# The first batch of an attention phase: another order of projections, gates and token splits

## The chip, the cores and the metric

The kernel runs on one NeuronCore of one Trainium2 chip. The metric is the device time of one execution in microseconds (us). The core has five engines with a queue of instructions each: TensorE (PE, matrix products into PSUM), VectorE (DVE), ScalarE (ACT), GpSimd (POOL) and SyncE (SP, here only DMA issues). Each queue runs in order; semaphores tie the queues together.

## The reference, cut to what matters

Eight batches of 576 tokens pass through linear attention and an MLP (the first phase, three quarters of the time) and then through a small mixture of attention experts (the second phase), of which this is the whole computation for a batch `x` (576 x 512):

```python
logits = x @ w_gate                              # 4 experts
topk = the two largest; w = softmax over those two
for e in range(4):
    q, k, v = x @ wq[e], x @ wk[e], x @ wv[e]     # head width 64
    scores = q @ k.T / 8, causal mask
    a = softmax(scores)
    out += (w of e where e is chosen, else 0) * (a @ v @ wo[e])
```

## The kernel before, in words

Every fp32 operand of a projection is split into a high part that TensorE multiplies fast (`hi`, a rounding cast) and the rest (`lo = x - hi`), and each product is three: hi*hi, lo*hi, hi*lo. So `Y[n]` holds a batch's tokens as `y_hi` and `y_lo`, alternately in two buffers, and each PSUM result that is an operand again is taken out twice: ScalarE casts the high part (`fill_hi`), then VectorE subtracts (`fill_lo`).

A batch of the second phase has these pieces of work:

- `("M", m)`, m = 0..7: the queries and keys of expert pair `p = m // 4` and half `h` of the sequence (`project_m`, 12 products, 256 columns wide for h = 0 and 320 for h = 1). m even is queries, odd is keys.
- `("V", t)`, t = 0..4: values and gate logits of a tile of 128 tokens (`project_v`, 12 products of 260 columns). ScalarE copies the values, VectorE the logits.
- 18 units (`UNITS`), 9 per expert pair: one head by 128 queries. `scores(n)` makes two units, and is called for two such pairs at steps 0, 4, 9 and 13, and alone at 8 and 17. `masked` (VectorE) adds the mask, writes the row to SBUF and finds the row maximum (`nmax`); `exponentials` (ScalarE) follows; `over_sum` (VectorE, L1351 and L1353) inverts the row sums; `scale` (GpSimd) multiplies by that and the gate; `turn_blocks` (VectorE, L1358) transposes blocks; `write_turned` (SP, four DMAs) and `land` (issued by ScalarE, which first waits for those four) carry the result through memory; `weighted` (TensorE) multiplies with the values.
- `("OUT", t)`: the product with `wo`, in the next batch.
- gates: `gates(st, shift, part)`, parts 0, 1 and 2 on VectorE (2, 6 and 10 small instructions), an exponential on ScalarE between (`gate_exp`).
- the split of the tokens two batches ahead: `load_y` (SP), `split_y` (GpSimd: four high parts and four low parts, alternating).

All engines walk the same 18 steps of a batch in their own queue, each doing its part of the step. `FILL` says which projection TensorE does in step n as filling between scores, `WEIGH` in which step `weighted` stands (steps from 18 on belong to the next batch), `TWOS` how units are grouped in twos. A step's fill goes to one of two PSUM banks (`bank(n)`), so it waits until the fill two before has been taken out (`fill_before`, `evacuated`). `scores(n)` waits for the maxima of the units that had its bank before: `scores(0)` of a batch waits for unit 16 of the batch before, `scores(2)` for unit 17.

Before step 0 of the very first batch there is a list, `ORDER0`: V0 to V3, M0 to M3, V4. The first batch then fills M4 to M7 (steps 0 to 3), V0 to V4 of batch 1 (4 to 8), M0 (9), M1, M2, M3 of batch 1 (15 to 17). Its gates stand in steps 0, 1 and 2, the gates of batch 1 in steps 14, 15 and 17 (`GATES_AT`). GpSimd makes batch 1's tokens (`split_y(.., 1, n)`) before its step 0, those of batch 2 from step 5 on, and splits `wo` in step 13 (L818, L820). VectorE's queue in a step is written out so:

```python
if n < UNITS and second(n, last):
    masked(st, n, first, last)
if fill_at(n - 1, first, last):
    fill_lo(...)
if n < UNITS and not second(n, last):
    masked(st, n, first, last)
```

and after these `sums_lo`, `over_sum` for the two units that began at n - 1, `turn_blocks` for those that began at n - 3, and the gates.

Of the kernel before, what the change touches and what calls it, by code (L numbers as in the profile page):

```python
# [5 lines left out]
ALU = mybir.AluOpType  # L6
# [10 lines left out]
def plain(ap):  # L17

    return ap.bitcast(F32)


def program(nc, q, k, v, g_ln, w_ch1, w_ch2, w_gate, wq, wk, wv, wo, out):
# [35 lines left out]
    with ExitStack() as ctx:  # L58
# [203 lines left out]
        for n in range(NT):  # L262
            FILL[4 + n] = ("V", n)
            FILL[10 + n] = ("OUT", n)

        WEIGH = {11: [(0, 0)], 17: [(0, 1)], UNITS + 2: [(1, 0)], UNITS + 8: [(1, 1)]}

        TWOS = [[p * NS + u for u in us] for p in range(EP) for us in ((0, 1), (2, 3), (4, 5), (6, 7), (8,))]
# [7 lines left out]

        def fill_at(n, first, last):

            if n == -1:
                return None if first else (("M", 3), 0)  # L280
            f = FILL.get(n)
            if f is None or (f[0] == "OUT" and first) or (last and (f[0] == "V" or (f[0] == "M" and f[1] < 4))):
                return None
            return f, {"OUT": -1, "V": 1, "M": 0 if f[1] >= 4 else 1}[f[0]]

        def fill_before(n, first, last):

            for at in range(n - 2, -1, -2):
                if fill_at(at, first, last):
                    return fill_at(at, first, last)  # L290
            return ((("M", 3), ("V", NT - 1))[n % 2] if first else ("M", 2 + n % 2)), 0

# [31 lines left out]

        def weighed(n, first, last):
            if last:
                own = [(w, 0) for w in WEIGH_LAST.get(n, [])]
            else:
                own = [(w, 0) for w in WEIGH.get(n, [])] if n < UNITS else []
            return own + ([] if first else [(w, -1) for w in WEIGH.get(n + UNITS, [])])  # L330

# [63 lines left out]

        ORDER0 = [("V", 0), ("V", 1), ("V", 2), ("V", 3), ("M", 0), ("M", 1), ("M", 2), ("M", 3), ("V", 4)]

# [19 lines left out]
        w2_in, wo_in_s = sem("w2_in"), sem("wo_in_s")  # L417
        w2s_hi, w2s_lo = sem("w2s_hi"), sem("w2s_lo")
        y0hi_a, y0lo_v, wo_g = sem("y0hi_a"), sem("y0lo_v"), sem("wo_g")
        y_ld = [sem(f"y_ld{kt}") for kt in range(KT)]  # L420
# [99 lines left out]
        def _(sp_):  # L520
# [153 lines left out]
            def batch(st, first=False, last=False, more=True):  # L674
                if more:
                    need2(sp_, "ylo_g", st, 1, KT)
                    load_y(st, 2)
                for n in range(UNITS):
                    f = fill_at(n - 1, first, last)
                    if f and f[0][0] == "OUT":  # L680
                        out_store(st, -1, f[0][1])
                    for k, shift in twos_at(n, 3, first, last):
                        if not (last and shift == 0):
                            write_turned(st, shift, k)
# [17 lines left out]
        def _(pool):  # L702
# [74 lines left out]
            def split_y(st, shift, n):  # L777
# [7 lines left out]
                else:  # L785
                    need2(pool, "yhi_g", st, shift, kt + 1)
                    pool.tensor_tensor(to[1][:, kt, 0:S], y_in[:, kt, :], plain(to[0][:, kt, 0:S]), ALU.subtract).then_inc(sems["ylo_g"], 1)

            def scale(st, shift, k, last):

                turn = last and shift == 0
                if k == 0:
                    need2(pool, "gate_v", st, shift, PER["gate_v"])
                need2(pool, "rrec_v", st, shift, 2 * k + 2)
                if not turn:
                    nth = nth_turned(st, shift, k)
                    if nth >= 4:
                        pool.wait_ge(px_out[nth % 4], 64 * (nth // 4))
                for i, u in enumerate(units_of(k, turn)):
                    p, s = unit(u, turn)  # L800
                    t = TILES_OF[s]
                    x = to = PR[s][:, 0 : P * t]
                    if not turn:

                        x = x.rearrange("p (j b c) -> p j b c", b=4, c=32)
                        to = PX[nth % 4][:, 0 : blocks_of(k)].rearrange("p (b x) -> p b x", b=4)[:, :, i * t * 32 : (i + 1) * t * 32].rearrange("p b (j c) -> p j b c", c=32)
                    g = G[(st[1] + shift) % 2][:, p, s : s + 1]
                    pool.tensor_scalar(to, x, rrec[:, 1, u : u + 1], g, ALU.mult, ALU.mult).then_inc(sems["pscale_g"], 1)  # L808

            def batch(st, first=False, last=False, more=True):  # L810
                for n in range(UNITS + 1 if last else UNITS):
                    for k, shift in twos_at(n, 2, first, last):
                        scale(st, shift, k, last)
                    if more and 5 <= n < 5 + 2 * KT:
                        split_y(st, 2, n - 5)
                    if first and n == 13:
                        pool.wait_ge(wo_in_s, 16 * E)
                        pool.tensor_tensor(WO[0][:], wo_in[:], ones[:, 0:1].rearrange("p (a c) -> p a c", a=1).to_broadcast([P, EP, D]), ALU.mult).then_inc(wo_g, 1)  # L818
                        pool.wait_ge(wo_g, 1)
                        pool.tensor_tensor(WO[1][:], wo_in[:], plain(WO[0][:]), ALU.subtract).then_inc(wo_g, 1)  # L820

            pool.sem_inc(sems["yhi_g"], KT)
            pool.sem_inc(sems["ylo_g"], KT)
            for n in range(2 * KT):
                split_y((0, 0), 1, n)
            batch((0, 0), first=True)
# [7 lines left out]
        def _(act):  # L834
# [135 lines left out]
            def gate_exp(st, shift):  # L970
                need2(act, "gate_v", st, shift, 2)
                act.activation(gate[:], gate[:], ACT.Exp).then_inc(sems["gexp_a"], 1)

            def exponentials(st, n, last):
                s = unit(n, last)[1]
                w = keys_of(s)
                need2(act, "nmax_v", st, 0, n + 1)
                act.activation(PR[s][:, 0:w], PR[s][:, 0:w], ACT.Exp, bias=nmax[:, n : n + 1], scale=-1.0, accum_out=rsum[:, n : n + 1]).then_inc(sems["exp_a"], 1)  # L978

            def batch(st, first=False, last=False):  # L980
                for n in range(STEPS_LAST if last else UNITS):
                    if n < UNITS and second(n, last):
                        exponentials(st, n, last)
                    if fill_at(n - 1, first, last):
                        f, shift = fill_at(n - 1, first, last)
                        fill_hi(st, shift, f, bank(n - 1))
                    for w, shift in weighed(n - 1, first, last):
                        sums_hi(st, shift, w, first, last and shift == 0)
# [11 lines left out]
                    if n < UNITS and not second(n, last):  # L1000
                        exponentials(st, n, last)
                    if n == 0 and first:
                        gate_exp(st, 0)
                    if n == GATES_AT[1] and not last:
# [5 lines left out]
            for i, f in enumerate(ORDER0):  # L1010
                if i == 1:
                    need(act, "y_v", (PAIRS, 0), KT)
                    act.copy(Y[0][0][:, :, CW:S], ysb[:, 0, :, 0:TAIL]).then_inc(y0hi_a, 1)
                if f == ("M", 0):
                    act.wait_ge(const2_g, 2)
                fill_hi((0, 0), 0, f, bank0(i))
            batch((0, 0), first=True)
            for n in range(1, 5):
# [8 lines left out]
        def _(dve):  # L1027
# [356 lines left out]
            def batch(st, first=False, last=False):  # L1384
                for n in range(STEPS_LAST if last else UNITS):
                    if n < UNITS and second(n, last):
                        masked(st, n, first, last)
                    if fill_at(n - 1, first, last):
                        f, shift = fill_at(n - 1, first, last)
                        fill_lo(st, shift, f, bank(n - 1))  # L1390
                    if n < UNITS and not second(n, last):
                        masked(st, n, first, last)
                    for w, shift in weighed(n - 1, first, last):
                        sums_lo(st, shift, w, last and shift == 0)
                    for k, shift in twos_at(n, 1, first, last):
                        over_sum(st, shift, k, last)
                    for k, shift in twos_at(n, 3, first, last):
                        if not (last and shift == 0):
                            turn_blocks(st, shift, k)
                    if first and n < 3:  # L1400
                        gates(st, 0, n)
                    if not last and n in GATES_AT:
# [17 lines left out]
            dve.wait_ge(const2_v, 1)  # L1420
            dve.wait_ge(const2_g, 13)
            batch((0, 0), first=True)
            for n in range(1, 5):
# [6 lines left out]
        def _(pe):  # L1430
# [251 lines left out]
            def batch(st, first=False, last=False):  # L1682
                for n in range(STEPS_LAST if last else UNITS):
# [5 lines left out]
                    if last and lagging(n, T_LAG, True, last):  # L1689
                        transposes(st, lagging(n, T_LAG, True, last)[0])  # L1690
                    for w, shift in weighed(n, first, last):
                        weighted(st, shift, w, first and shift == 0, last and shift == 0)
                    if fill_at(n, first, last):
                        f, shift = fill_at(n, first, last)
                        what, x = f
                        held, when = fill_before(n, first, last)
                        evacuated(st, when, held)
# [21 lines left out]
            for i, f in enumerate(ORDER0):  # L1719
# [5 lines left out]
                if i == 0:  # L1725
                    pe.wait_ge(y0lo_v, KT)
                if f == ("M", 2):
                    pe.wait_ge(y0lo_v, KT + 1)
                if f == ("V", NT - 1):
                    pe.wait_ge(const2_v, 1)  # L1730
# [37 lines left out]
```

## Time and profile before

| | |
|---|---|
| median of three runs | 1256.91 us (1255.25 to 1259.26) |
| the profiled execution: its own time | 1256.5 us |
| its span, first to last instruction | 1254.7 us |
| mean granted TensorE clock | 0.995 of full |
| second phase, from its first projection | 891.6 us on |
| first batch, steps 0 to 17 | about 905 to 948 us |

The rows below give a start in us from the beginning of the span and a duration. A clock of 1.00 is TensorE's level of 2.4 GHz, a stretch of about 0.5 is its level of 1.2 GHz.

### The profile page before, as it was taken

The numbers are of one execution on the slowest core, as the hardware profiler recorded it, in microseconds if no ns is written. First come the engines' busy times: TensorE is split into PE (matmuls) and PEld (weight loads), VectorE is DVE, ScalarE is ACT, GpSimd is POOL, SyncE is SP. The second block draws the span as 40 slices with busy tenths as digits, with TensorE's granted clock in tenths as the row PEclk, the third lists the DMA queues.
The fourth block names the chain that finished last, engine by engine and source line by source line (L and its number), as shares of the span: only waits on it lengthen the run. The fifth ranks groups of instructions, "written<-read, shape, count | busy, mean of one in ns | idle before, by whom it ended". The sixth has DMA issues, their size and how long they took to land.

```text
span 1254.7 us, 19440 instructions
## 1 busy us (share of the span) xinstructions
PE 1223.0 (97%) x7136; PEld 1016.7 (81%) x7136; DVE 668.7 (53%) x1750; ACT 379.5 (30%) x858; POOL 224.3 (18%) x252
## 2 busy tenths in 40 slices
PE   8989999999999999999999999999988999999998
PEld 7878888888888888888888888888977788878876
DVE  5785365465365375365365313311476666666652
ACT  4462131131131131131131111111334455445545
POOL 3532000000000000000000000001474455445321
PEclk9999999999999999999999999999989999999989
DMA  8741550550460360370370130250356777786742
GB/s 183 179 105 46 130 78 9 124 86 5 121 95 5 107 110 5 103 112 5 92 123 5 45 90 7 67 112 1 89 149 175 222 207 209 220 234 195 188 128 76
DMA packets 344735, 133.05 MB, mean 106 GB/s; under 512 B 240960, under 2 KB 329024, under 8 KB 344640
## 3 DMA queue, kind: packets, MB, share of 16 engines
q1 hardware_dynamic: 296400, 108.85, 36.3%
q10 hardware_dynamic: 48240, 22.94, 7.3%
q8 instruction: 58, 0.95, 0.3%
q14 instruction: 37, 0.30, 0.1%
HBM read 72.10 MB, written 42.86 MB: 92 GB/s over the span
## 4 chain that ended last, share of the span: by engine, by line
PE 79%; DVE 9%; DMA 3%; ACT 3%; SPq 3%; issue 2%; ACTq 0%; POOL 0%; DVEq 0%; POOLq 0%
PE hb L1434 31%; PE yb L1522 30%; PE sc L1434 9%; PE pa L1451 3%; DMA turned<-px 3%; PE ob L1678 2%; DVE px L1358 2%; ACT prob L978 1%; SPq L672 1%; DVE prob L1376 1%; PE pa L1442 1%; PE sc L1644 1%; SPq L531 1%; DVE k_lo L1295 1%; DMA vsb<-in_v_dram 0%
## 5 line engine op out<-in xcount | busy, mean ns | idle before, releaser
L1228 DVE SCALAR_TENSOR_TENSOR hid_lo<-hb,hid_hi 128x512 fp32r<-128x512 f32 x144 | 99.4, 690 | 383.3 <-ACT hid_hi L868 383.3
L868 ACT ACTIVATE hid_hi<-hb 128x512 fp32r<-128x512 f32 x144 | 85.8, 597 | 614.8 <-PE hb L1434 614.8
L1522 PE MATMUL yb<-hid_hi,w_hi 128*128 128x512 f32 x576 | 226.5, 393 | 2.4 <-DVE hid_lo L1228 2.4
L1434 PE MATMUL hb<-xn_hi,w_hi 128*128 128x512 f32 (+1 forms) x580 | 228.2, 393 | 0.0
L1434 PE MATMUL hb<-xn_lo,w_hi 128*128 128x512 f32 (+1 forms) x580 | 225.2, 388 | 0.0
L1434 PE MATMUL hb<-xn_hi,w_lo 128*128 128x512 f32 (+1 forms) x580 | 225.0, 388 | 0.0
L1522 PE MATMUL yb<-hid_hi,w_lo 128*128 128x512 f32 x576 | 224.3, 389 | 0.0
L1522 PE MATMUL yb<-hid_lo,w_hi 128*128 128x512 f32 x576 | 224.1, 389 | 0.0
L1434 PEld LDWEIGHTS hb<-xn_hi,w_hi 128*128 128x128 f32 x580 | 108.9, 188 | 25.7 <-issue 2.3
L1522 PEld LDWEIGHTS yb<-hid_hi,w_hi 128*128 128x128 f32 x576 | 108.1, 188 | 24.9 <-issue 2.8
L1434 PEld LDWEIGHTS hb<-xn_hi,w_lo 128*128 128x128 f32 x580 | 108.9, 188 | 22.8
L1522 PEld LDWEIGHTS yb<-hid_hi,w_lo 128*128 128x128 f32 x576 | 108.1, 188 | 22.8
L1434 PEld LDWEIGHTS hb<-xn_lo,w_hi 128*128 128x128 f32 x580 | 109.0, 188 | 21.3
L1522 PEld LDWEIGHTS yb<-hid_lo,w_hi 128*128 128x128 f32 x576 | 108.2, 188 | 21.7
L978 ACT ACTIVATE prob<-prob,nmax 128x128 f32<-128x128 f32 (+3 forms) x144 | 84.0, 584 | 124.8 <-DVE nmax L1376 109.6
L808 POOL TENSOR_SCALAR px<-prob,rrec,g 128x128 f32<-128x128 f32 (+4 forms) x126 | 79.5, 640 | 146.1 <-DVE rrec L1353 130.4
L716 POOL TENSOR_TENSOR vsb<-ones 128x40 f32<-128x40 f32 x8 | 2.4, 306 | 507.6 <-PE hb L1434 507.6
L1434 PE MATMUL sc<-y_hi,wqk_hi 128*128 128x256 f32 (+1 forms) x256 | 79.5, 310 | 8.3 <-DVE k_lo L1295 4.8
L1434 PE MATMUL sc<-y_lo,wqk_hi 128*128 128x256 f32 (+1 forms) x256 | 75.8, 296 | 0.0
L1434 PE MATMUL sc<-y_hi,wqk_lo 128*128 128x256 f32 (+1 forms) x256 | 75.8, 296 | 0.0
L1434 PEld LDWEIGHTS sc<-y_hi,wqk_hi 128*128 128x128 f32 x256 | 48.7, 190 | 14.0 <-DVE k_lo L1295 6.2
L1358 DVE STREAM_TRANSPOSE px<-px 128x256 f32<-128x256 f32 (+4 forms) x70 | 57.9, 828 | 0.0
(221 smaller groups left out, 1853.1 us busy)
## 6 DMA issues: line engine op xcount, KB each, us to landing
qx<-in_q_dram SPq DMA_DIRECT2D x32, 288.0 KB, 5.5
ksb<-in_k_dram SPq DMA_DIRECT2D x8, 1024.0 KB, 5.7
vsb<-in_v_dram SPq DMA_DIRECT2D x32, 256.0 KB, 4.8
stage<-in_moe_w_ch_dram SPq DMA_DIRECT2D x16, 512.0 KB, 3.9
xn_lo<-ksb SPq DMA_DIRECT2D x128, 64.0 KB, 2.0
y_scratch<-ysb SPq DMA_DIRECT2D x32, 256.0 KB, 2.9
ysb<-xsb SPq DMA_DIRECT2D x128, 64.0 KB, 2.1
out_dram<-osb SPq DMA_DIRECT2D x32, 256.0 KB, 4.2
```

The lines of the kernel that those rows point to most:

```text
L531: sp_.dma_start(qx[b * 32 : (b + 1) * 32], q_v[st[1], st[0], b // 2, b % 2]).then_inc(q_in, 16)
L672: sp_.dma_start(to[a], PX[nth % 4][a * 32 : (a + 1) * 32, 0 : 4 * w].rearrange("c (b x) -> c b x", b=4)).then_inc(px_out[nth % 4], 16)
L808: pool.tensor_scalar(to, x, rrec[:, 1, u : u + 1], g, ALU.mult, ALU.mult).then_inc(sems["pscale_g"], 1)
L868: act.activation(HID[f % 2][0][:], hb[f % 2][:], ACT.Relu).then_inc(sems["hhi_a"], 1)
L978: act.activation(PR[s][:, 0:w], PR[s][:, 0:w], ACT.Exp, bias=nmax[:, n : n + 1], scale=-1.0, accum_out=rsum[:, n : n + 1]).then_inc(sems[" ...
L1228: dve.scalar_tensor_tensor(out=lo[:], in0=hb[f % 2][:], scalar=0.0, in1=plain(hi[:]), op0=ALU.max, op1=ALU.subtract).then_inc(sems["hlo_v" ...
L1295: dve.tensor_tensor(K[1][:, p, s0 * HQ : s1 * HQ], src[:, 0 : CHUNK[h]], plain(K[0][:, p, s0 * HQ : s1 * HQ]), ALU.subtract).then_inc(sems ...
L1358: dve.transpose(x, x).then_inc(sems["px_v"], 1)
L1434: ins = pe.matmul(dst, l, r, start=(n == 0), stop=(n == len(terms) - 1))
L1451: ins = pe.matmul(dst[r, X_BANK[g], g % 2 * 2 * (HD + 1) : (g % 2 + 1) * 2 * (HD + 1)], qx[:, g, 4 * t : 4 * t + ROWS[t] // 32, :], KV[:, ...
L1522: ins = pe.matmul(yb[j][:], l, r, start=(f == 0 and m == 0 and not first), stop=(f == FT - 1 and m == 2), skip_group_check=True)
L1678: ins = pe.matmul(OB[nth % 2][e * HD : (e + 1) * HD, at : CHUNK[h]].rearrange("p (a c) -> p a c", c=32), v[:, j, 2 * p + e, :], PT[h][:, a ...
```

## The change

`ORDER0` becomes M0, M1, V0 to V4. The first batch gets tables of its own: M2 and M3 in steps 0 and 1, M4 to M7 in 2 to 5, V0 to V4 of batch 1 in 6 to 10, M0 and M1 of batch 1 in 11 and 12, M2 and M3 in 16 and 17. The weighted sums of its second half of queries (0, 1) move from step 17 to step 1 of batch 1. Gates parts 0 and 1 stand before step 0, part 2 in step 1 ahead of the fill. The high parts of batch 1's tokens are cast by ScalarE (`y1_hi`: one before the batch, three in steps 0 to 2), GpSimd does the low parts only (`y1_lo`: one before, two in step 2, one in step 4). GpSimd's split of batch 2's tokens starts in step 9, the split of `wo` moves to step 17, and SP's loads of batch 2's tokens go to step 4.

```diff
+        FILL_FIRST = {n: (("M", 2 + n), 0) for n in range(6)}
+        FILL_FIRST.update({6 + n: (("V", n), 1) for n in range(NT)})
+        FILL_FIRST.update({(11, 12, 16, 17)[n]: (("M", n), 1) for n in range(4)})
+
         WEIGH = {11: [(0, 0)], 17: [(0, 1)], UNITS + 2: [(1, 0)], UNITS + 8: [(1, 1)]}
+        WEIGH_FIRST = {11: [(0, 0)], UNITS + 1: [(0, 1)], UNITS + 2: [(1, 0)], UNITS + 8: [(1, 1)]}
...
-            return ((("M", 3), ("V", NT - 1))[n % 2] if first else ("M", 2 + n % 2)), 0
+            return (("V", 3 + n % 2) if first else ("M", 2 + n % 2)), 0
...
-        ORDER0 = [("V", 0), ("V", 1), ("V", 2), ("V", 3), ("M", 0), ("M", 1), ("M", 2), ("M", 3), ("V", 4)]
+        ORDER0 = [("M", 0), ("M", 1), ("V", 0), ("V", 1), ("V", 2), ("V", 3), ("V", 4)]
...
             def batch(st, first=False, last=False, more=True):
-                if more:
-                    need2(sp_, "ylo_g", st, 1, KT)
-                    load_y(st, 2)
                 for n in range(UNITS):
+                    if more and n == (4 if first else 0):
+                        need2(sp_, "ylo_g", st, 1, KT)
+                        load_y(st, 2)
...
+            def y1_lo(kt):
+
+                pool.wait_ge(y1hi_a, kt + 1)
+                pool.tensor_tensor(Y[1][1][:, kt, 0:S], y_in[:, kt, 0:S], plain(Y[1][0][:, kt, 0:S]), ALU.subtract).then_inc(sems["ylo_g"], 1)
...
-                    if more and 5 <= n < 5 + 2 * KT:
-                        split_y(st, 2, n - 5)
-                    if first and n == 13:
+                    if first and n in (2, 4):
+                        for kt in ((1, 2), (3,))[n // 4]:
+                            y1_lo(kt)
+                    at = n - (9 if first else 5)
+                    if more and 0 <= at < 2 * KT:
+                        split_y(st, 2, at)
+                    if first and n == UNITS - 1:
...
-            for n in range(2 * KT):
-                split_y((0, 0), 1, n)
+            y1_lo(0)
...
+            def y1_hi(kt):
+                act.wait_ge(y_ld[kt], 32)
+                act.copy(Y[1][0][:, kt, 0:S], y_in[:, kt, 0:S]).then_inc(y1hi_a, 1)
...
-                    if n == 0 and first:
-                        gate_exp(st, 0)
+                    if first and n < KT - 1:
+                        y1_hi(n + 1)
...
+            y1_hi(0)
+            gate_exp((0, 0), 0)
+            act.wait_ge(const2_g, 2)
             batch((0, 0), first=True)
...
                         masked(st, n, first, last)
+                    if first and n == 1:
+                        gates(st, 0, 2)
...
-                    if first and n < 3:
-                        gates(st, 0, n)
...
+            gates((0, 0), 0, 0)
+            gates((0, 0), 0, 1)
             batch((0, 0), first=True)
```

## Rows read from the trace of the kernel before

**Rows 1.** The page's first line: the span.

```profile
span 1254.7 us, 19440 instructions
```

**Rows 2.** Windows: stretch, length, busy time (PE, PEld, DVE, ACT, POOL), TensorE clock, DMA.

```profile
905.20:918.00 12.80, 10.52 (x74) 9.05 (x73) 9.01 (x37) 5.47 (x17) 7.28 (x7) 0.87 0.28 93
914.50:918.50 4.00, 4.00 (x21) 2.92 (x20) 2.57 (x14) 1.59 (x6) 1.24 (x3) 0.57 0.48 173
918.00:954.70 36.70, 28.88 (x217) 24.96 (x217) 27.68 (x92) 14.85 (x48) 24.80 (x26) 0.95 0.60 157
...
954.70:1207.50 252.80, 248.97 (x1835) 209.42 (x1836) 168.51 (x639) 124.69 (x386) 119.18 (x150) 1.00 0.74 207
```

**Rows 3.** The chain that ended last: the second phase's first projections (V0, V1).

```profile
891.58 2.89 PE ob L1434 x24
```

**Rows 4.** TensorE's timeline: the first instruction of ten pieces; idle before, releaser.

```profile
897.21 0.28 PE L1434 MATMUL sc<-y_hi,wqk_hi 128*128 128x256 f32 x1
...
900.03 0.31 PE L1434 MATMUL sc<-y_hi,wqk_hi 128*128 128x320 f32 x1
...
903.56 0.39 PE L1434 MATMUL sc<-wvg_hi,y_hi 128*128 128x260 f32 x1
...
906.09 0.39 PE L1434 MATMUL sc<-y_hi,wqk_hi 128*128 128x256 f32 x1
...
913.13 0.42 PE L1434 MATMUL sc<-y_hi,wqk_hi 128*128 128x320 f32 x1 [2.28 <-DVE k_lo L1295]
...
917.91 0.47 PE L1434 MATMUL sc<-wvg_hi,y_hi 128*128 128x260 f32 x1
...
933.68 0.50 PE L1644 MATMUL sc<-k_hi,q_hi 64*128 64x512 f32 x2 [2.36 <-DVE nmax L1376]
...
941.56 2.27 PE L1678 MATMUL ob<-pt,v 128*64 128x320 f32 x20 [1.23 <-DMA pt<-turned]
...
946.38 0.41 PE L1434 MATMUL sc<-y_hi,wqk_hi 128*128 128x320 f32 x1 [2.55 <-DVE k_lo L1295]
...
958.41 0.44 PE L1644 MATMUL sc<-k_hi,q_hi 64*128 64x384 f32 x2
```

**Rows 5.** Timeline of GpSimd and VectorE: two pairs that overlap.

```profile
910.33 1.43 POOL L787 TENSOR_TENSOR y_lo<-y_in,y_hi 128x576 fp32r<-128x576 f32 x1
...
910.53 1.33 DVE L1327 TENSOR_TENSOR gcmp<-gcmp,before 128x80 f32<-128x80 f32 x1
...
939.10 2.43 POOL L820 TENSOR_TENSOR wo_lo<-wo_in,wo_hi 128x1024 fp32r<-128x1024 f32 x1
...
939.95 1.62 DVE L1323 TENSOR_TENSOR gate<-logit,gmx 128x20 f32<-128x20 f32 x1
```

**Rows 6.** VectorE's timeline: V4's logits, gates (first and last), two of the masks.

```profile
905.71 0.16 DVE L1307 COPY logit<-sc 128x4 f32<-128x4 f32 x1 [1.01 <-ACT v L936]
...
909.29 1.06 DVE L1325 TENSOR_TENSOR gcmp<-logit 128x80 f32<-128x80 f32 x1
...
912.44 0.17 DVE L1330 TENSOR_SCALAR grank<-grank 128x20 f32<-128x20 f32 x1
...
913.33 0.17 DVE L1333 TENSOR_TENSOR gate<-gate,grank 128x20 f32<-128x20 f32 x1
...
914.47 0.67 DVE L1343 COPY g<-gate 32x2 f32<-32x2 f32 x4
...
928.49 0.29 DVE L1376 CUSTOM_DVE_ANT_0 prob<-tb,mask 128x128 f32<-128x128 f32 x1
...
944.06 0.69 DVE L1376 CUSTOM_DVE_ANT_0 prob<-sc,mask 128x512 f32<-128x512 f32 x1
```

**Rows 7.** ScalarE's timeline: four token casts, a pair of query casts, an exponential.

```profile
886.67 2.17 ACT L1009 CAST y_hi<-y_in 128x512 fp32r<-128x512 f32 x4
...
902.26 0.42 ACT L932 CAST qt_hi<-sc 64x64 fp32r<-64x64 f32 x2
...
907.50 0.39 ACT L978 ACTIVATE prob<-prob,nmax 128x128 f32<-128x128 f32 x1
```

More of the change, by code:

```diff
@@ L275, in program, with fill_at @@
         STEPS_LAST = UNITS + 5
-        def fill_at(n, first, last):
+        def fill_at(n, st, first, last):
             if n == -1:
                 return None if first else (("M", 3), 0)
+            if first:
+                f = FILL_FIRST.get(n)
+                return None if f is None else f
             f = FILL.get(n)
@@ L284, in fill_at, with fill_before @@
             return f, {"OUT": -1, "V": 1, "M": 0 if f[1] >= 4 else 1}[f[0]]
-        def fill_before(n, first, last):
+        def fill_before(n, st, first, last):
             for at in range(n - 2, -1, -2):
-                if fill_at(at, first, last):
-                    return fill_at(at, first, last)
-            return ((("M", 3), ("V", NT - 1))[n % 2] if first else ("M", 2 + n % 2)), 0
+                if fill_at(at, st, first, last):
+                    return fill_at(at, st, first, last)
+            return (("V", 3 + n % 2) if first else ("M", 2 + n % 2)), 0
         def lagging(n, lag, first, last):
@@ L323, in landing, with weighed @@
             return PT[h][:, at : at + (4 if u == NS - 1 else 8), 0:t, :]
-        def weighed(n, first, last):
+        def weighed(n, st, first, last):
             if last:
@@ L328, in weighed @@
             else:
-                own = [(w, 0) for w in WEIGH.get(n, [])] if n < UNITS else []
-            return own + ([] if first else [(w, -1) for w in WEIGH.get(n + UNITS, [])])
+                own = [(w, 0) for w in (WEIGH_FIRST if first else WEIGH).get(n, [])] if n < UNITS else []
+            return own + ([] if first else [(w, -1) for w in (WEIGH_FIRST if st[1] == 1 else WEIGH).get(n + UNITS, [])])
         def unit(n, turn):
@@ L418, in program @@
         w2s_hi, w2s_lo = sem("w2s_hi"), sem("w2s_lo")
+        y1hi_a = sem("y1hi_a")
         y0hi_a, y0lo_v, wo_g = sem("y0hi_a"), sem("y0lo_v"), sem("wo_g")
@@ L674, in batch @@
             def batch(st, first=False, last=False, more=True):
-                if more:
-                    need2(sp_, "ylo_g", st, 1, KT)
-                    load_y(st, 2)
                 for n in range(UNITS):
-                    f = fill_at(n - 1, first, last)
+                    if more and n == (4 if first else 0):
+                        need2(sp_, "ylo_g", st, 1, KT)
+                        load_y(st, 2)
+                    f = fill_at(n - 1, st, first, last)
                     if f and f[0][0] == "OUT":
@@ L820, in batch @@
                         pool.tensor_tensor(WO[1][:], wo_in[:], plain(WO[0][:]), ALU.subtract).then_inc(wo_g, 1)
-            pool.sem_inc(sems["yhi_g"], KT)
+            pool.sem_inc(sems["yhi_g"], 2 * KT)
             pool.sem_inc(sems["ylo_g"], KT)
-            for n in range(2 * KT):
-                split_y((0, 0), 1, n)
+            y1_lo(0)
             batch((0, 0), first=True)
@@ L983, in batch @@
                         exponentials(st, n, last)
-                    if fill_at(n - 1, first, last):
-                        f, shift = fill_at(n - 1, first, last)
+                    if fill_at(n - 1, st, first, last):
+                        f, shift = fill_at(n - 1, st, first, last)
                         fill_hi(st, shift, f, bank(n - 1))
-                    for w, shift in weighed(n - 1, first, last):
+                    for w, shift in weighed(n - 1, st, first, last):
                         sums_hi(st, shift, w, first, last and shift == 0)
@@ L1013, in _ @@
                     act.copy(Y[0][0][:, :, CW:S], ysb[:, 0, :, 0:TAIL]).then_inc(y0hi_a, 1)
-                if f == ("M", 0):
-                    act.wait_ge(const2_g, 2)
                 fill_hi((0, 0), 0, f, bank0(i))
+            y1_hi(0)
+            gate_exp((0, 0), 0)
+            act.wait_ge(const2_g, 2)
             batch((0, 0), first=True)
@@ L1387, in batch @@
                         masked(st, n, first, last)
-                    if fill_at(n - 1, first, last):
-                        f, shift = fill_at(n - 1, first, last)
+                    if first and n == 1:
+                        gates(st, 0, 2)
+                    if fill_at(n - 1, st, first, last):
+                        f, shift = fill_at(n - 1, st, first, last)
                         fill_lo(st, shift, f, bank(n - 1))
@@ L1392, in batch @@
                         masked(st, n, first, last)
-                    for w, shift in weighed(n - 1, first, last):
+                    for w, shift in weighed(n - 1, st, first, last):
                         sums_lo(st, shift, w, last and shift == 0)
@@ L1690, in batch @@
                         transposes(st, lagging(n, T_LAG, True, last)[0])
-                    for w, shift in weighed(n, first, last):
+                    for w, shift in weighed(n, st, first, last):
                         weighted(st, shift, w, first and shift == 0, last and shift == 0)
-                    if fill_at(n, first, last):
-                        f, shift = fill_at(n, first, last)
+                    if fill_at(n, st, first, last):
+                        f, shift = fill_at(n, st, first, last)
                         what, x = f
-                        held, when = fill_before(n, first, last)
+                        held, when = fill_before(n, st, first, last)
                         evacuated(st, when, held)
@@ L1726, in _ @@
                     pe.wait_ge(y0lo_v, KT)
-                if f == ("M", 2):
+                if f == ("V", NT - 1):
                     pe.wait_ge(y0lo_v, KT + 1)
-                if f == ("V", NT - 1):
                     pe.wait_ge(const2_v, 1)
```

## The prediction

> **What bounds the kernel now.** I read the views from the outside in. The profiled execution took 1256.5 us, of which 1254.7 are its span [rows 1] and 1.8 lie around it; the median of the runs, 1256.91, is 0.4 above it. The change touches only the second phase's first batch, so I cut the phase into windows [rows 2]. From 954.70 to 1207.50 TensorE is busy 248.97 of 252.80 us at full clock, and the change leaves that stretch's instructions alone: whatever the first batch saves or loses arrives at the end undiminished. In the first batch and the start of the second, TensorE stands still 12.80 - 10.52 = 2.3 us and 36.70 - 28.88 = 7.8 us, and its clock is short by 12.80 x 0.13 = 1.7 and 36.70 x 0.05 = 1.8 us. That makes 13.6 us, the most that any order can win.
>
> TensorE's timeline says whom it waited for [rows 4]: VectorE, three times out of four. Once it is a low part that stood behind the gates (M7 at 913.13, 2.28 us late, after which the clock fell to 0.57 for 4 us [rows 2]), once a row maximum (933.68, 2.36), once a low part again (946.38, 2.55), and once a DMA (941.56, 1.23). So the question for each edit is what it does to VectorE's queue.
>
> **The opening.** Before, V0 starts at 891.58 [rows 3], and four V take until 897.21: 1.41 each. M0 and M1 take 900.03 - 897.21 = 2.82, M2 and M3 903.56 - 900.03 = 3.53, V4 and the first two scores 2.53 together, and M4 starts at 906.09 [rows 4]. After, the order is M0, M1, five V, scores, M2, M3: the same work, so M4 could start at 906.1 again. What changes is when VectorE and ScalarE get their input: scores(0) starts at 891.58 + 2.82 + 5 x 1.41 = 901.5, about 3.5 us earlier.
>
> M4 needs M2's bank, so M2's low part. Before it on VectorE stand, from V4's logits on, gates parts 0 and 1, two masks and part 2. V4's logits were there 905.87 - 903.56 = 2.3 after V4's start [rows 4, 6]; after, that is 900.05 + 2.3 = 902.3. Part 0 is two instructions of the kind of L1330 and L1333 (0.2 each with the gap): 0.4. Part 1 took 912.61 - 909.29 = 3.3 before [rows 6], in which L1325 (1.06) and L1327 (1.33) are far above their neighbours of about 0.2; without these excesses it is 1.3 to 1.4. Here it meets the first `y1_lo` on GpSimd, 1.43 us [rows 5]. I take 902.3 + 0.4 + 1.3 + 1.4 = 905.4 (904.0 without the meeting). Two masks of 0.3, then part 2, 915.14 - 913.33 = 1.8 [rows 6]: 907.9. On ScalarE from 905.8: exp(0) 0.5 with its read-out, `y1_hi(1)` 2.17 / 4 = 0.54 for 512 columns, so 0.6 for 576, exp(1) 0.5, M2's casts 0.3 + 0.4 [rows 7]: 908.1. Then VectorE's low part of M2 with its turned queries, 0.8: M4 starts near 909.1, 3.0 us later than before, and the clock falls as it did after the 2.28 us. From M4 to V0 of batch 1 TensorE had 917.91 - 906.09 - 2.28 - 1.7 = 7.9 us of work; with one clock loss of 1.7 again, V0 starts at 909.1 + 7.9 + 1.7 = 918.7 against 917.91. So the old stall before M7 is not removed: it moves ahead to M4 and grows a little, because two thirds of the gates stand in front of the first maxima instead of between them. Loss here 0.8; if gates meet no GpSimd instruction, gain 0.6.
>
> **Token work.** Four high parts leave GpSimd for ScalarE, 0.6 us each on an engine that is busy 5.47 of 12.80 us [rows 2]; their cost is only the one or two that stand before M2's casts, counted above. If ScalarE had no slack, all four would cost 2.4. The last low part follows scale(1) in step 4, near 916, ahead of V0's 918.7; that is its cover, 2 us. SP's loads of batch 2 wait for it and then finish near 922; GpSimd wants them in step 9, near 925.
>
> **Steps 6 to 17.** TensorE runs V0 to V4, scores and M0, M1 of batch 1 nearly without a wait. With S(9) two fills earlier, the mask of unit 9 comes at 928.49 - 2 x 1.4 + 0.8 = 926.5 or a little before: 926.0 to 926.5. From here VectorE's and ScalarE's chain of maxima, exponentials, sums and transposes governs. Before, it took from 928.49 to 944.06, 15.6 us, for units 9 to 16 [rows 6]. After, it holds in addition a logit and a low part (0.5), and the neighbours on GpSimd differ. A VectorE instruction with SBUF operands only that meets a GpSimd instruction ends when that ends: L1327 at 911.86 behind `y_lo` at 911.76, L1323 at 941.57 behind `wo_lo` at 941.53 [rows 5], where their like take 0.2. The change lays GpSimd's eight token splits into steps 9 to 16, that is beside the gates of batch 1 (steps 14, 15), where before only `wo` stood. I expect three meetings on the path, of 1.1 to 1.4 by these rows, 3.7 in all: L1351, and L1326 and L1328 or their neighbours. The stretch before holds such meetings too (L1323's 1.4 is in its 15.6), so the net is between -3.7 (none is left) and +4.7 (below); I add 0.7, half a meeting. So unit 16's maximum is there at 926.2 + 15.6 + 0.5 + 0.7 + 0.7 (its own time) = 943.7.
>
> The Trainium skill, page "SBUF — State Buffer", section "Who interferes with whom", states it as a rule: a VectorE instruction with two SBUF inputs and a GpSimd instruction that reads SBUF exclude each other for the whole instruction, while ScalarE waits for neither. The trace agrees with the first half, as the two pairs above show. By the rule the casts moved to ScalarE are free of it; had the meetings shared the port instead of excluding each other, the maximum would come about 3 us sooner.
>
> TensorE has no work until then. Clean work from V0 to the common point (scores(4) of batch 1, 958.41 [rows 4]) is 958.41 - 917.91 - 7.8 - 1.8 = 30.9 us. Of it 10.4 stand behind scores(0) of batch 1: scores 0.9, M4 to M7 2.82 + 3.53, the moved sums (0, 1) 2.27, and (1, 0) at 8/20 of that, 0.9. So TensorE is through at 918.7 + 20.5 = 939.2 and waits 4.5 us for unit 16 at 943.7, then 3.1 for unit 17 at 947.2 (exp(16) 0.8, M2's two casts and two subtractions 1.5, transposes 0.9, the mask 0.7, less overlap). The moved sums would have filled this, but they now stand behind the wait; their old DMA wait of 1.23 and the 2.55 before M3 are gone. From 947.2 remain 10.0 us of work and one clock loss of 1.7: scores(4) at 958.9, 0.5 later than before.
>
> **The sum.** Losses after: 3.0 and 4.5 + 3.1 of standing still and twice 1.7 of clock, 14.0, against 13.6 before, so about +0.5. Carried forward piece by piece with the same durations, the order of before reaches 960.7 where the trace has 958.41, and the order of after 959.5; like for like this says -1.2. I take a value between, nearer to the second: -0.9 from the median, 1256.0. Nothing later changes it [rows 2]. The split of `wo` in step 17, whose second half takes 2.43 [rows 5], holds up gates part 2 at most that long; behind these on VectorE wait M3's low part and the first masks of batch 1, and M4 and the sums (0, 1), 3.7 us, cover it. Uncovered it costs up to 2.4.
>
> **Rivals.**
> - *The meetings stay away (faster).* VectorE's gates fall between GpSimd's instructions. For it: part 2 of the first gates, ten instructions in 1.8 us [rows 6], ran without a meeting. Against: GpSimd's scale is released by `over_sum`, and the splits follow at once, so they return beside the same VectorE instructions. Unit 16 comes 3.7 earlier: 1252.3. Chance 0.19. Less than 941 for scores(0) of batch 1 decides it.
> - *Every wait of the first batch goes (faster still).* The work is there; against it is all of VectorE's queue. -9 to -13: 1246. Chance 0.03.
> - *Every port-bound instruction of the gates meets one (slower).* Part 0, part 1 and L1351 have seven; each 1.2 is 8.4 instead of the 3.7 on the path: +4.7, 1260.7. GpSimd has four splits in that stretch, 1.43 or a little less each, the scales between and `wo` after it, so the supply is there. Chance 0.10. It decides if scores(2) of batch 1 start after 951.
> - *The opening goes as meant* (M4 without a wait): 4.7 us are won by V0, but the chain of maxima starts only as much earlier as VectorE is free, and the clock stays up: 1253 to 1255, inside the forecast's range. It is a part of the forecast's case.
>
> **How the numbers follow.** Forecast as told: 0.68. About 0.3%, 3.8 us, is what a measurement of this kernel tells from no change, so faster means under 1253.1 and slower over 1260.7. Faster 0.22 is the sum of the first two rivals; slower 0.10; same 0.68. The range reaches to 1251.0, which leaves about 1 in 10 of the faster cases and the 1246 outside, and up to 1260.3, short of the slower rival.
>
> **What would show it.** M4 of the first batch starts near 909 with about 3 us of idle time, released by M2's low part (`qt_lo`), and a clock near 0.57 in the next 4 us; V0 of batch 1 near 918.7. No stall over 1 us between 919 and 938. Then one stall of 3 to 5 us and one of 2 to 4 before scores(0) and scores(2) of batch 1, released by `nmax`, with L1323, L1326 or L1328 over 1 us beside `y_hi`, `y_lo`. Scores(4) of batch 1 within 956 to 961. The forecast is wrong if the scores of batch 1 start without a wait, or if the chain of maxima is short enough in its own right.

## The result, and the profile after

The changed kernel takes 1260.97 us (median of 14 runs, 1256.62 to 1262.35), the kernel before 1257.03 (14 runs, 1254.92 to 1260.51). The ratio is 1.0029, with a 95% interval of 1.0018 to 1.0040: slower, by 3.9 us in the medians. That is 0.7 us above the range. The prediction put the bound of "slower" at about 0.3%, or 1260.7 us: the median is just over the second, the ratio just under the first.

The profiled execution after has a span of 1260.3 us, 5.6 more than before. Its second phase starts 1.2 us later (892.77 instead of 891.58, [rows 3]) in a stretch that the change does not touch, so 4.4 are the phase's own. I count times from that first projection below ("+x"). The windows of after, with the columns of [rows 2]:

```profile
905.20:918.00 12.80, 10.28 (x76) 9.48 (x75) 8.92 (x41) 7.56 (x26) 6.46 (x8) 1.00 0.05 11
918.00:954.70 36.70, 22.96 (x172) 20.34 (x171) 26.77 (x84) 12.63 (x40) 23.36 (x24) 0.85 0.66 183
954.70:970.00 15.30, 15.30 (x113) 12.92 (x112) 7.75 (x29) 5.98 (x20) 4.00 (x7) 0.92 0.52 131
```

The second window holds the loss: TensorE is idle for 13.7 us instead of 7.8, at a mean clock of 0.85 instead of 0.95. The low clock reaches into the third window (0.92). The steady batches behind it are as full as before: from 970.00 to 1215.00 TensorE is busy 241.05 of 245.00 us, at 1.00. TensorE's timeline after, first instructions of six pieces, against [rows 4]:

```profile
892.77 0.28 PE L1459 MATMUL ob<-y_hi,wqk_hi 128*128 128x256 f32 x1
...
910.11 0.39 PE L1459 MATMUL sc<-y_hi,wqk_hi 128*128 128x256 f32 x1 [2.52 <-DVE qt_lo L1325]
...
918.48 0.39 PE L1459 MATMUL sc<-wvg_hi,y_hi 128*128 128x260 f32 x1
...
951.90 0.47 PE L1669 MATMUL sc<-k_hi,q_hi 64*128 64x128 f32 x2 [10.65 <-POOL wo_lo L839]
...
956.34 2.70 PE L1703 MATMUL ob<-pt,v 128*64 128x320 f32 x20
...
965.09 0.44 PE L1669 MATMUL sc<-k_hi,q_hi 64*128 64x384 f32 x2
```

One row stands out: scores(0) of batch 1 waited 10.65 us, and the releaser is not VectorE's maximum but GpSimd's split of `wo`. In the code that is `pe.wait_ge(wo_g, 2)`, which stands in TensorE's queue between the first batch and the loop over batches 1 to 4 (line 1737 of the kernel before). It cost nothing while the split was made in step 13: [rows 5] have it done at 941.53, and scores(0) of batch 1 started about 948. In step 17 it is behind scale(8). VectorE and GpSimd after, with the meetings (a VectorE instruction that lies beside one of GpSimd and ends when that ends):

```profile
904.06 1.43 POOL L802 TENSOR_TENSOR y_lo<-y_in,y_hi 128x576 fp32r<-128x576 f32 x1 [11.42 <-ACT y_hi L994]
...
904.15 1.43 DVE L1348 TENSOR_TENSOR gcmp<-logit 128x80 f32<-128x80 f32 x1
...
940.59 1.11 DVE L1348 TENSOR_TENSOR gcmp<-logit 128x80 f32<-128x80 f32 x1
...
941.88 1.32 DVE L1350 TENSOR_TENSOR gcmp<-gcmp,before 128x80 f32<-128x80 f32 x1
...
943.99 0.69 DVE L1399 CUSTOM_DVE_ANT_0 prob<-sc,mask 128x512 f32<-128x512 f32 x1
...
947.52 0.76 DVE L1399 CUSTOM_DVE_ANT_0 prob<-tb,maskt 128x576 f32<-128x576 f32 x1
...
948.20 1.26 DVE L1356 TENSOR_TENSOR gate<-gate,grank 128x20 f32<-128x20 f32 x1
...
949.51 2.34 POOL L839 TENSOR_TENSOR wo_lo<-wo_in,wo_hi 128x1024 fp32r<-128x1024 f32 x1
...
949.71 2.16 DVE L1358 TENSOR_SCALAR gmx<-gmx 128x5 f32<-128x5 f32 x1
```

Unit 16's maximum was there at 944.7 and unit 17's at 948.3. Without the wait, scores(0) could have started at 944.7 and scores(2) at 948.3, where they came at 951.9 and 952.6.

### The profile page after: what moved, and what is told of

Same layout as the page of the kernel before. It is cut to its first block, busy times and chain, and to the rows that moved or that the text cites. A ratio compares the mean times of both kernels' runs of the same rounds, so it can differ in the third digit from the quotient of the medians.

```text
span 1260.3 us, 19439 instructions
## 1 busy us (share of the span) xinstructions
PE 1222.0 (97%) x7136; PEld 1017.4 (81%) x7136; DVE 670.2 (53%) x1750; ACT 382.1 (30%) x862; POOL 220.4 (17%) x248
## 4 chain that ended last, share of the span: by engine, by line
PE 77%; DVE 9%; DMA 4%; ACT 3%; SPq 3%; issue 2%; POOL 1%; ACTq 1%; DVEq 0%; POOLq 0%
PE hb L1459 31%; PE yb L1547 30%; PE sc L1459 7%; DMA turned<-px 3%; PE pa L1476 3%; PE ob L1703 2%; DVE px L1381 2%; SPq L682 2%; ACT prob L1000 1%; PE pa L1467 1%; DVE prob L1399 1%; SPq L541 1%; ACTq L986 1%; DVE k_lo L1318 1%; PE sc L1669 1%
## 5 line engine op out<-in xcount | busy, mean ns | idle before, releaser
L1459 PE MATMUL sc<-y_hi,wqk_hi 128*128 128x320 f32 (+1 forms) x248 | 77.2, 311 | 6.5 <-DVE qt_lo L1325 2.5
L1459 PE MATMUL sc<-y_lo,wqk_hi 128*128 128x320 f32 (+1 forms) x248 | 73.3, 296 | 0.0
L1459 PE MATMUL sc<-y_hi,wqk_lo 128*128 128x320 f32 (+1 forms) x248 | 73.3, 296 | 0.0
```

What stands on the lines that cost most here:

```text
L1459: ins = pe.matmul(dst, l, r, start=(n == 0), stop=(n == len(terms) - 1))
```

## The experiments

All ratios are to the kernel before, run in the same group of runs on the same chip, with their 95% intervals. The groups are e1 to e4 (kernel before 1256.75 us), e5 to e8 (1255.96), and e9 and e10 (1256.25). The kernel before differs by up to 0.8 us between groups, so across groups the ratios count and not the medians. Each kernel has 11 or 12 runs, e10 only 6.

**e1: the wait alone.** TensorE waits for `wo` where it is first read.

```diff
             batch((0, 0), first=True)
-            pe.wait_ge(wo_g, 2)
             for n in range(1, 5):
...
                         else:
+                            if x == 0 and st == (0, 1):
+                                pe.wait_ge(wo_g, 2)
                             output(st, shift, x, bank(n), 4 if x == 0 else 0)
```

> The changed kernel with one wait moved: TensorE waits for the split of wo ahead of the first product with wo (step 10 of batch 1), no longer ahead of batch 1's scores(0). Theory (the wait is the loss): scores(0) of batch 1 then start when unit 16's maximum is there, at 944.7 instead of 951.9 in the trace of after, scores(2) at 948.3 instead of about 952.4; the end moves forward by 3 to 4.5 us, so about 1256.5 where the changed kernel has 1261, level with the kernel before or up to 1 us under it. Rival (the wait hides behind VectorE): gates part 2 of batch 1 lasts until 953.1 beside the split of wo and stands ahead of M3's low part and the masks, so TensorE stops at M5 instead and the end moves by less than 1 us: 1260 to 1261.

Measured: 1256.28 us, ratio 0.9991 (0.9978 to 1.0004). The whole loss is gone, with all the rest of the change in place, as the theory had it. TensorE's timeline of e1 (its first projection is at 893.30):

```profile
944.04 0.33 PE L1669 MATMUL sc<-k_hi,q_hi 64*128 64x128 f32 x2 [3.79 <-DVE nmax L1399]
...
947.54 0.58 PE L1669 MATMUL tb<-k_hi,q_hi 64*128 64x256 f32 x2 [2.75 <-DVE nmax L1399]
```

The two stalls that the prediction had (4.5 and 3.1) are here, 3.79 and 2.75, both for row maxima; M5 did not stall. Scores(0) come at +50.7 instead of +59.1 after, scores(4) of batch 1 (959.70) at +66.4 instead of +72.3; before it was +66.8. Of the 8.4 us that scores(0) gain, 5.9 are left at scores(4), in part because the stall before scores(2) is back. The rival, that VectorE's gates part 2 would hold TensorE up as long, is refuted.

A caution for single profiles: the mask that finds unit 16's maximum starts at +51.2 in the changed kernel, +49.9 in e1 and +50.0 in e5, whose instructions are the same up to there. So differences of up to 1.3 us in such a place are scatter, and the medians decide.

**e2: the split of `wo` back in step 13**, the wait where it was (`if first and n == UNITS - 1:` becomes `n == 13`).

> The changed kernel with the split of wo back in step 13; TensorE's wait stays where it was. Theory (the late split is the loss): no wait for GpSimd at batch 1, but 4.3 us of split ahead of scale(7) and between token splits, beside VectorE's gates: 1257 to 1259, so most of the loss gone. Rival (port meetings of VectorE with GpSimd are the loss, the wait only covers them): the meetings in steps 14 and 15 become more, unit 16's maximum comes later than 944, and the time stays at 1260 to 1262.

Measured: 1256.87 us, 1.0003 (0.9989 to 1.0017). The loss is gone this way too, the time a shade under the theory's 1257. The rival (meetings, not the wait) is out: there are more meetings here (L1346 takes 1.62 us beside `wo_lo`), and the loss is gone all the same. They may cost something: scores(0) of batch 1 wait 5.19 us for their maximum and stand at +53.1, 2.4 us after e1's, more than the scatter.

**e3: the kernel before with this one part of the change**, the split of `wo` in step 17.

> The kernel before with one part of the change alone: the split of wo in step 17 instead of 13. Theory (TensorE's wait at the head of batch 1 for a split in step 17): scale(7) ends near 948 there, wo near 952.5, TensorE waits for it from about 948 on, the end is 2 to 4.5 us later: 1259.5 to 1261.5. Rival (the loss comes of the new order, not of wo): within 1 us of the kernel before, 1256 to 1258, because VectorE's queue is relieved in steps 14 and 15 by as much.

Measured: 1259.00 us, 1.0017 (1.0001 to 1.0034). One line gives part of the loss in the old order, half a microsecond less than I had expected at the least, and the interval all but reaches 1. The timeline of e3, in which the split ends at 950.02:

```profile
950.07 0.33 PE L1644 MATMUL sc<-k_hi,q_hi 64*128 64x128 f32 x2 [4.15 <-POOL wo_lo L820]
```

The wait is 4.15 us here and 10.65 in the changed kernel, since there TensorE had been through with steps 16 and 17 long before, and the weighted sums (0, 1) stood behind the wait instead of in front of it. Part of it is paid back: M3's stall is 0.65 in e3, 2.55 before [rows 4].

**e4: the split of `wo` in step 6**, the wait where it was (`n == 6`).

> The changed kernel with the split of wo in step 6, where GpSimd stands idle for 1.8 and 2.7 us around its scales; the wait stays. Theory (late split is the loss): no wait for GpSimd at batch 1, gates part 2 without the meetings of 1.3 and 2.2 us: 1255.5 to 1257.5, the best of these four, since unit 16's maximum stays at 944 to 945. Rival (VectorE's meetings in steps 14 to 17 and its chain are the loss): scores(0) of batch 1 still late by 3 us or more against its chain, 1259 or more.

Measured: 1256.80 us, 0.9999 (0.9986 to 1.0012): in the theory's range, with the rival's 1259 or more out, but not the best of the four. Gates part 2 took its short form (L1356 and L1358 0.17 us each); the meetings of part 1 stayed (L1348 1.10, L1350 1.32), so scores(0) of batch 1 still waited 3.60 and scores(2) 2.96 for maxima, and the split in step 6 delayed the units behind it: scores(11) waited 1.67.

**e5: the moved sums between the two scores.** e1, with `weighted(0, 1)` behind scores(0) of batch 1 and ahead of scores(2). The call is skipped where it stood before; that line is left out here.

```diff
-        WEIGH_FIRST = {11: [(0, 0)], UNITS + 1: [(0, 1)], ...
+        WEIGH_FIRST = {11: [(0, 0)], UNITS: [(0, 1)], ...
...
                         scores(st, n, first, last)
+                        if st == (0, 1) and n == 0:
+                            weighted(st, -1, (0, 1), False, False)
                         if not last and n % NS < NS - 1:
                             scores(st, n + 2, first, last)
```

> The changed kernel with TensorE's wait for wo at its first use, and the moved weighted sums (0, 1) between scores(0) and scores(2) of batch 1 instead of behind both. Theory (TensorE's idle time at the head of batch 1 can be filled by them, only their place behind the wait kept them out): the stall before scores(2), 2.75 us with the wait moved alone, shrinks to about 0.4 and the end comes 1.5 to 2.3 us sooner than that kernel's 1256.3, so 1254 to 1255. Rival (VectorE decides there: gates part 2, lengthened by the split of wo, stands before M3's low part, for which M5 waits): the idle time only moves to M5, 1256 to 1256.5.

Measured: 1254.87 us, 0.9990 (0.9978 to 1.0002), against e1's 0.9991: no difference that these runs can tell, as the rival had it. The median as such lies in the theory's range (1254 to 1255), but that is the faster group and no gain on e1. The trace sides with the rival: the stall before scores(2) (2.75) is gone, new ones of 2.40 before M5 and 0.60 before M6 stand in its place, and scores(4) come at +66.5, where e1 has +66.4. M5 waits for M3's low part behind gates part 2:

```profile
950.73 0.39 PE L1459 MATMUL sc<-y_hi,wqk_hi 128*128 128x256 f32 x1 [2.40 <-DVE k_lo L1318]
```

**e6: the first batch's gates back in steps 0, 1 and 2**, on e1: the calls of `gates` and `gate_exp` as in the kernel before.

> The changed kernel with the wait for wo at its first use, and the first batch's gates back in steps 0, 1 and 2. Theory A (the gates ahead of the first masks cause the 2.5 us stall before M4, but the chain of maxima in steps 9 to 17 decides the end): M4 starts with under 1 us of idle time, a stall of 1 to 2.5 comes back before M6 or M7, and the end stays within 1 us of 1256.3. Theory B (the opening's stall and its clock loss are paid in full): 1252.5 to 1254.5.

Measured: 1257.27 us, 1.0015 (1.0001 to 1.0029). Theory B is out: without the 2.5 us stall before M4 (0.76 here) nothing was won. Theory A's end came true, just (1.0 us above 1256.3), but not its stall of 1 to 2.5 before M6 or M7: small ones came instead (0.60, 0.39, 0.88, and later 1.27). Scores(0) of batch 1 stand at +52.7, 2.0 later than in e1, not much beyond the scatter. The intervals of e6 and e1 overlap by a hair, so that gates ahead of the first masks help a little is likely, not certain.

**e7: the token splits of batch 2 three steps earlier**, on e1 (`at = n - (6 if first else 5)`).

> The changed kernel with the wait for wo at its first use, and GpSimd's split of batch 2's tokens in steps 6 to 13 instead of 9 to 16. Theory (VectorE's gate instructions of batch 1 are held up by these splits, 1.1 and 1.3 us at L1348 and L1350): both take about 0.24 us, unit 16's maximum and scores(0) of batch 1 come 1.5 to 2.2 us sooner, the end 1 to 2.2 us sooner: 1254 to 1255.3. Rival (the waiting time is only moved: over_sum and others meet the splits in the steps before, and ScalarE's waits for the DMAs set the pace): L1348 and L1350 short, but the same end within 0.7 us of 1256.3.

Measured: 1253.06 us, 0.9976 (0.9966 to 0.9986): faster than the kernel before. The median is 0.9 under the theory's range; by the ratios the gain on e1 is 0.15% or 1.9 us, which is in it. The intervals of e7 and e1 overlap (0.9978 to 0.9986), so a gain on e1 is likely, not certain. The rows that the theory named, VectorE and TensorE of e7 (first projection at 890.78):

```profile
938.27 0.24 DVE L1348 TENSOR_TENSOR gcmp<-logit 128x80 f32<-128x80 f32 x1
...
938.69 0.24 DVE L1350 TENSOR_TENSOR gcmp<-gcmp,before 128x80 f32<-128x80 f32 x1
```

```profile
940.57 0.33 PE L1669 MATMUL sc<-k_hi,q_hi 64*128 64x128 f32 x2 [1.42 <-DVE nmax L1399]
```

The same instructions took 1.10 and 1.32 us in e1. Of these 2.0 us, 0.9 arrive at scores(0) (+49.8 against +50.7) and at scores(4) (+65.5 against +66.4), which is within the scatter; scores(2) still wait 2.95. Two more profiles have the early splits, e9 and e10. In e7, e9 and e10 the mask of unit 16 starts at +49.0, +47.9 and +48.3, in the changed kernel, e1 and e5 at +51.2, +49.9 and +50.0. So the maximum does come earlier, by about 1 us at the least.

How much of that reaches the end is not settled, for two other things differ by as much. The mean granted clock over e7's twelve runs is 0.9948, over e1's 0.9927: over 1250 us that is 2.6 us more at full speed. And in the profiles the stretch behind scores(4) of batch 1, in which e1 and e7 have the same instructions, takes 297.5 us in e1 and 294.4 in e7.

**e8: three edits together**, on e1: the sums of e5, the gates of e6, the split of `wo` in step 8.

> A candidate: the changed kernel with the wait for wo at its first use, the sums (0, 1) between scores(0) and scores(2) of batch 1, the first batch's gates back in steps 0 to 2, and the split of wo in step 8. If the idle stretches add up as the single edits suggest: 1252.5 to 1254.5, faster than both kernels. If the chain of maxima through steps 9 to 17 decides alone: 1255.5 to 1256.5.

Measured: 1255.20 us, 0.9994 (0.9979 to 1.0008), between the two ranges and near the second; the single edits do not add up: scores(0) of batch 1 waited 4.49 us for unit 16's maximum, and the sums could not fill that, since they stand behind it.

**e9: `wo` without the port meeting.** e7, and ScalarE casts `wo`'s high part in step 3, GpSimd makes the low part in step 4.

```diff
+                    if first and n == 3:
+                        act.wait_ge(wo_in_s, 16 * E)
+                        act.copy(WO[0][:], wo_in[:]).then_inc(wo_g, 1)
...
-                    if first and n == UNITS - 1:
+                    if first and n == 4:
                         pool.wait_ge(wo_in_s, 16 * E)
-                        pool.tensor_tensor(WO[0][:], wo_in[:], ...
                         pool.wait_ge(wo_g, 1)
```

> A candidate on top of the kernel with the wait at its first use and the token splits in steps 6 to 13: ScalarE casts the high part of wo in step 3, GpSimd makes only its low part, in step 4. Theory (gates part 2 of batch 1 is held up 1.0 and 2.0 us by the split of wo at L1356 and L1358; behind it wait M3's low part and the masks of batch 1): part 2 takes 1.8 us instead of 5, but M5 of batch 1 was covered by M4 and the sums (0, 1), so the end moves little: 1252 to 1253.5, within 1 us of that kernel's 1253.1. Rival (part 2 was on the path of batch 1's maxima): 1250.5 to 1251.5.

Measured: 1254.39 us, 0.9986 (0.9976 to 0.9996). The rival is out. Gates part 2 is short (L1358 and L1360, the lines that were L1356 and L1358, take 0.18 and 0.17 us), and the end does not move forward for it, as expected of something that TensorE's other work had covered. Against e7 it is if anything 1 us worse, inside the intervals, and 0.9 us above the theory's range.

**e10: e9 with the sums of e5.**

> The same candidate with the sums (0, 1) between scores(0) and scores(2) of batch 1. With gates part 2 short, M5 no longer waits for it, so the 2.3 us of sums should now fill the stall of 2.95 before scores(2) for good: 1.5 to 2.3 us under the same kernel without this edit, 1250 to 1251.5. Rival (some later wait takes it back, as in the kernel with this edit alone, where M5 waited 2.4 us): within 0.7 us of it.

Measured: 1251.98 us, 0.9969 (0.9955 to 0.9982), 2.4 us under e9 in the medians of the same group. The gain is slightly more than the theory's 1.5 to 2.3; the time itself is 0.5 us above its 1251.5. All six runs lie under e9's median. It is the fastest kernel of this study, 4.3 us under the kernel before and, by the ratios, about 7.5 under the changed one. TensorE of e10 (first projection at 892.41):

```profile
941.52 0.33 PE L1671 MATMUL sc<-k_hi,q_hi 64*128 64x128 f32 x2 [1.42 <-DVE nmax L1401]
...
945.03 0.39 PE L1671 MATMUL tb<-k_hi,q_hi 64*128 64x256 f32 x2 [0.75 <-DVE nmax L1401]
```

Scores(4) of batch 1 (954.03) are at +61.6, 5.2 us ahead of the kernel before and 3.3 ahead of e9 (+64.9). Of these 3.3 us, 2.2 are the shorter stall, less a new one of 0.60 before M6. The rest, 1.7, goes with the clock, which in this stretch stayed up in e10 only (e9 first, then e10; clock in the third column from the end):

```profile
942.00:950.00 8.00, 5.05 (x25) 4.00 (x26) 6.63 (x27) 3.27 (x13) 2.40 (x3) 0.57 0.75 224
942.00:950.00 8.00, 6.93 (x60) 5.14 (x58) 6.56 (x27) 3.53 (x14) 2.40 (x3) 1.00 0.74 225
```

The same sums between the scores were worth nothing in e5 and 2.4 us here: in e5 gates part 2, stretched by the split of `wo`, took the time back at M5.

## Why the prediction was wrong

**The step that failed** stands at the end of the sum: "The split of `wo` in step 17 ... holds up gates part 2 at most that long ... and M4 and the sums (0, 1), 3.7 us, cover it. Uncovered it costs up to 2.4." I asked who waits behind VectorE, and did not ask who waits for the split itself. TensorE does, at the head of batch 1, in front of M4 and the sums that I had named as the cover. In the trace of before that wait leaves no row, because the split ends 7 us ahead of it; only the queue in the code shows it. In the changed kernel it ran until 951.9, 7.2 us after unit 16's maximum and 3.6 after unit 17's. e1 moves this wait alone and gives 0.9991 instead of 1.0029, 4.8 us, twice the "up to 2.4". Its 1256.3 is close to the 1256.0 that I had forecast with the wait overlooked, but closer than the terms deserve: they missed by 1 to 3 us each, on both sides (below). e2 and e4 take the same loss away from the other side, and e3 puts 0.17% (0.01 to 0.34) of it into the kernel before.

The same step also mis-sized what it did look at. Gates part 2 met both halves of the split, L1356 beside `wo_hi` and L1358 beside `wo_lo`, and lost 3.1 us to them where I had "at most" 2.4. M4 and the sums covered that in e1, where M5 did not wait; in e5, with the sums moved away, they did not (2.40 before M5).

**The other steps**, against the trace after, with its 1.2 us of offset taken off:

- The opening: M4 at 908.9 (forecast 909.1) with 2.52 us idle (3.0), released by M2's turned queries as named. V0 of batch 1 at 917.3 (918.7); the clock loss of 1.7 that I had charged did not come in this execution (window clock 1.00). Where it came, V0 was 1.0 us later, not 1.7 (last section). The meeting of gates part 1 with the first `y1_lo` is there, L1348 at 1.43 us. But e6 shows that this stall is no loss that the end sees, so counting it in full did no harm only because I took the later chain as the governing one.
- Token work on ScalarE: no cost shows. V0 of batch 1, the row at 918.48 above, has no wait.
- Steps 6 to 17: stalls of 1.26, 0.33 and 1.22, where I had said none above 1. The maximum of unit 16 is there at 943.5 (943.7), of unit 17 at 947.1 (947.2). That close a hit is in part luck: unit 9's mask came 0.6 later than forecast (926.8), and the meetings cost less.
- The meetings: three were charged on the path, 3.7 us in all. Two came at L1348 and L1350 (before the change L1325 and L1327, the neighbours of the named L1326 and L1328), 1.11 and 1.32 long, 1.9 more than their like; L1374 (the `over_sum` instruction) took 0.56 and 0.39 instead of 0.17. That is 2.6 us in all. e7 takes the first two away.
- TensorE out of work at the head of batch 1: confirmed, 3.79 and 2.75 us in e1, where 4.5 and 3.1 were forecast, with one clock loss behind them.
- "The moved sums would have filled this": true, but e5 only moved the wait on to M5. It took e10, with gates part 2 short, to gain by it.
- The rivals: the time fell on the slower one's side, and even its sign came (scores(2) of batch 1 after 951), but by another mechanism. Its own, more port meetings, is refuted: they cost 2.6 us in the trace and not 8.4, and with them in place and the wait moved, e1 is level with the kernel before.

By the rule of the Trainium skill that was weighed, page "SBUF — State Buffer", section "Who interferes with whom", a GpSimd instruction that reads SBUF and a VectorE instruction with two SBUF inputs exclude each other. The traces agree: L1348 and L1350 took 1.10 and 1.32 us beside a split (e1, e4) and 0.24 each alone (e7). L1358, a scalar operation with one SBUF input of 5 columns, was also held up, for 2.0 us by `wo_lo`; the same section counts such operations in, where they run in a two-port mode.

What stays open: how much of e7's gain is the early splits and how much the clock, and why e9 is not faster than e7. Between these two the mean granted clock of the runs differs as well (0.9933 and 0.9948, 1.9 us over 1250); what moved it is not shown. The order of gates and masks in the opening (e6) is settled only in sign, and weakly.

## What to carry to other kernels

When a producer is moved later, search the code for every wait on its semaphore, on every engine, and ask where in its queue each stands: a wait that cost nothing has no row in the trace, and its place at the head of a loop, not at the first use, turned a hidden split into 10.65 us of idle time. Put such a wait where the data is read. Work meant to fill a stall must stand ahead of the wait in its queue, and it pays only when the next wait behind it is gone as well: the same edit gave nothing that could be told in e5, and 2.4 us in e10. When a forecast lands near the measured time, check its terms one by one: here several missed, and the misses cancelled.

## What the runs showed of the hardware

The same idle time did not always cost TensorE's clock. The stall before M4 was 2.51 or 2.52 us in eight of these profiles. In the 10 us from 908.00 to 918.00 the mean granted clock was then 1.00 in four of them (after, e2, e7, e9) and 0.83 in the other four (e1, e4, e5, e10). I found nothing ahead of the stall that tells the two kinds apart: M4 starts at +17.3 in all eight. The row of e1, against the first window of after above:

```profile
905.20:918.00 12.80, 10.29 (x68) 9.49 (x67) 9.01 (x39) 7.67 (x23) 6.96 (x8) 0.87 0.06 12
```

So a clock loss behind a stall of this length came in half of these executions, and a sum should carry it as a range. It also cost less than 0.17 of 10 us, or 1.7: V0 of batch 1 starts at +26.7 or +26.8 in the four with the loss and at +25.7 in the four without, 1.0 us apart. Unit 16's mask is no later for it (+49.9 and +50.0 in e1 and e5, +51.2 after; +48.3 in e10, +47.9 in e9), so these profiles do not show it reaching the end.

At the head of batch 1, between 942 and 956, the granted clock fell to the lower level, 0.50 (1.2 GHz), in every profile with the new order but e10's, which has stalls of only 1.42 and 0.75 us there; it fell in e7 and e9 too, with stalls of 1.42 or 1.41 and 2.95. After the idle time of 10.65 us it was still low from 951.90 to 956.40, and the weighted sums (0, 1) take 2.70 us instead of the 2.27 of [rows 4].
